# Seven half-size products per pair of hidden chunks in a banded-attention + MLP kernel

## The reference

```python
k_sum = k.reshape(B, H, nb, block, D).max(axis=3)
v_sum = v.reshape(B, H, nb, block, D).mean(axis=3)
...
a = np.exp(scores_all)
a = a / (np.sum(a, axis=-1, keepdims=True) + 1e-09)
...
g = x @ w_gate
silu = g * (1.0 / (1.0 + np.exp(-g)))
val = x @ w_val
return (silu * val @ w_out).astype(np.float32)
...
h = x @ w_in
g = np.where(pos, h, np.where(neg, 0.0, (h + beta) ** 2 / (4.0 * beta)))
return (g @ w_out).astype(np.float32)
```

## Time and profile before

| | us |
|---|---|
| median of 3 runs | 649.57 |
| lowest, highest | 646.45, 650.25 |
| span of the profiled execution | 649.1 |
| TensorE busy in it | 627.6 |
| VectorE, ScalarE, GpSimd busy | 356.3, 323.3, 30.4 |

### The profile page before, as it was taken

One profiled execution on the slowest core, in us unless ns is written; L12 is line 12 of the kernel. 1 busy time (PEld: TensorE's weight loads), 2 busy tenths in 40 slices (PEclk: granted clock), 3 DMA queues, 4 the chain that ended last, 5 costly groups with the idle time before them and its releaser, 6 DMA issues.

```text
span 649.1 us, 9400 instructions
## 1 busy us (share of the span) xinstructions
PE 627.6 (97%) x3144; PEld 510.9 (79%) x3144; DVE 356.3 (55%) x553; ACT 323.3 (50%) x622; POOL 30.4 (5%) x33
## 2 busy tenths in 40 slices
PE   5779989999999999999999999999999999999997
PEld 2648868888888888888888888888888888888885
DVE  6855455544455555445333447666666666666664
ACT  1844576773468686434333344444444444444442
POOL 3310000100010101000000000000000000000000
PEclk9989979999999999999999999999999999999999
DMA  9997936512922221322332223232253332333221
GB/s 282 261 308 215 223 98 149 160 54 99 253 97 70 75 88 57 97 98 97 97 97 97 65 66 97 97 97 97 97 164 97 97 97 97 125 134 97 97 81 65
DMA packets 49780, 78.51 MB, mean 121 GB/s; under 512 B 16481, under 2 KB 21601, under 8 KB 49505
## 3 DMA queue, kind: packets, MB, share of 16 engines
q1 hardware_dynamic: 49760, 78.27, 39.8%
HBM read 72.48 MB, written 3.15 MB: 117 GB/s over the span
## 4 chain that ended last, share of the span: by engine, by line
PE 88%; SPq 5%; DMA 3%; DVE 1%; ACT 1%; issue 1%; DVEq 0%; ACTq 0%
PE bank L409 49%; PE bank L472 20%; PE bank L454 14%; DMA v_tok<-v_rows_dram 2%; PE bank L344 2%; PE bank L335 2%; SPq L207 2%; DMA win_raw<-w_dram 1%; SPq L203 1%; PE bank L328 1%; PE bank L321 1%; SPq L226 1%; DVE k_sum L681 1%; SPq L233 0%; ACT prob L536 0%
## 5 line engine op out<-in xcount | busy, mean ns | idle before, releaser
L409 PE MATMUL bank<-x_hi,win_hi 128*128 128x512 f32 (+1 forms) x480 | 191.6, 399 | 0.0
L409 PE MATMUL bank<-x_lo,win_hi 128*128 128x512 f32 (+1 forms) x480 | 188.1, 392 | 0.0
L409 PE MATMUL bank<-x_hi,win_lo 128*128 128x512 f32 (+1 forms) x480 | 187.8, 391 | 0.0
L593 ACT ACTIVATE hid_hi<-v_tok 128x512 fp32r<-128x512 f32 x84 | 53.0, 631 | 128.4 <-DVE v_tok L804 75.5
L409 PEld LDWEIGHTS bank<-x_lo,win_hi 128*128 128x128 f32 x480 | 90.7, 189 | 19.4
L409 PEld LDWEIGHTS bank<-x_hi,win_hi 128*128 128x128 f32 x480 | 90.7, 189 | 19.2 <-issue 0.2
L409 PEld LDWEIGHTS bank<-x_hi,win_lo 128*128 128x128 f32 x480 | 90.7, 189 | 18.3 <-issue 0.2
L774 DVE TENSOR_TENSOR hid_lo<-v_tok,hid_hi 128x512 fp32r<-128x512 f32 x84 | 65.5, 780 | 56.1 <-ACT hid_hi L593 56.0
L764 DVE TENSOR_TENSOR win_lo<-win_raw,win_hi 128x512 fp32r<-128x512 f32 (+1 forms) x84 | 76.9, 916 | 19.5 <-ACT win_hi L569 19.5
L472 PE MATMUL bank<-wout_hi,hid_hi 128*128 128x512 f32 x192 | 74.8, 389 | 0.3 <-ACT hid_hi L593 0.3
L472 PE MATMUL bank<-wout_hi,hid_lo 128*128 128x512 f32 x192 | 74.8, 390 | 0.0
(11 more groups left out here) (54 smaller groups left out, 576.4 us busy)
## 6 DMA issues: line engine op xcount, KB each, us to landing
wout_raw<-w_dram SPq DMA_DIRECT2D x84, 256.0 KB, 2.6
win_raw<-w_dram SPq DMA_DIRECT2D x36, 512.0 KB, 4.1
win_raw<-w_dram SPq DMA_DIRECT2D x48, 256.0 KB, 3.0
k_slot<-k_t_dram SPq DMA_DIRECT2D x24, 192.0 KB, 4.7
v_slot<-v_rows_dram SPq DMA_DIRECT2D x24, 192.0 KB, 5.2
v_tok<-v_rows_dram SPq DMA_DIRECT2D x4, 768.0 KB, 8.9
out_dram<-v_slot SPq DMA_DIRECT2D x12, 256.0 KB, 3.0
k_raw<-k_t_dram SPq DMA_DIRECT2D x2, 1056.0 KB, 12.1
```

The costliest lines, as they stand in the source:

```text
L409: last = nc.tensor.matmul(dst[:], a, m, start=k == 0 and i == 0, stop=k == KD - 1 and i == 2)
L593: nc.scalar.activation(hid_hi[:, r], hid[:, r], ACT.Copy).then_inc(hid_hi_ready, 1)
```

## The change

**Input projections.** The tokens are taken in two groups of 768, one batch each, and each group as two halves of 384 columns (`T`). A unit makes two hidden chunks at once, as a 2 x 2 block product: the weights' blocks A11, A12, A21, A22 (two chunks by two halves of the 512 inputs) and the tokens' blocks B11, B21, B12, B22. Instead of 8 block products it makes 7 (`p1` to `p7`), with sums of blocks as operands. The sums of weights (`weight_sums`: S1 to S4) are made on GpSimd for every unit, the sums of tokens (`x_sums`: T1 to T4) once for each phase on VectorE and GpSimd. Sums are split in hi and lo like the blocks. The four outputs C11, C12, C21, C22 share partial sums: one PSUM bank (`x_ps`) collects P1, then P6, P7 and P4 on top of each other, and ScalarE copies it out after each of the first three (`p1_copy`, `u2_copy`, `u3_copy`); a second (`v_ps`) collects P5 and P3. VectorE adds a copy to a bank for C11, C22 and C12 (`c11`, `c22`, `c12`). In layer 1 a gate unit and a value unit alternate; Silu is applied to the finished copies, and GpSimd (`gated`) and VectorE (`h21`) multiply.

**Phases.** There are four: layer 1 for group 0 and for group 1, layer 2 for group 0 and for group 1, with 12, 12, 8 and 8 units. All hidden units of a phase stay in SBUF (`h`), and the output projection of the phase follows as a part of its own: `out1`, 24 matmuls of 384 columns for each of 12 chunks into 8 banks, or `out2`, 18 matmuls of 512 columns for each of 16 chunks into 6 banks. During it the seven operands of the next phase are split (`x_part_hi`, `x_part_lo`) and, in layer 2, the activation is made chunk by chunk (`rel_of`, `hid_of`).

**Attention.** The 12 tiles of batch 0 run ahead of the MLP, the 12 of batch 1 one for each unit of phase 0. For those GpSimd subtracts the maximum (`shift`) and ScalarE makes one exponential for the tile; VectorE sums it. Outputs of a tile are copied as fp32 into `raw`.

**Buffers and loops.** Tiles lie at offsets written by hand, many on top of each other; raw weights have three buffers. `wout_lo` is made by GpSimd. There are no hardware loops left.

**TensorE**, input projection: before, a step of layer 1 is a row of these three, eight times over (`x_hi,win_hi` and so on are the two operands).

The diff, cut to its core:

```diff
-            def project(dst, r, c0, tok):
-
-                for k in range(KD):
-                    c = c0 + k * P
-                    w = (win_hi[:, r, c:c + P], win_lo[:, r, c:c + P])
-                    x = (x_hi[:, k, bass.ds(tok, TB)], x_lo[:, k, bass.ds(tok, TB)])
-                    for i, (a, m) in enumerate(passes(w, x)):
-                        last = nc.tensor.matmul(dst[:], a, m, start=k == 0 and i == 0,
-                                                stop=k == KD - 1 and i == 2)
-                return last
...
+T = S // 2
+PH_LEN = (CH1, CH1, CH2 // 2, CH2 // 2)
+PH_U0 = (0, CH1, 2 * CH1, 2 * CH1 + CH2 // 2)
+CH_LEN = (CH1, CH1, CH2, CH2)
+CH_N0 = (0, CH1, 2 * CH1, 2 * CH1 + CH2)
+PHASES = 4
+UNITS = PH_U0[-1] + PH_LEN[-1]
+RAWS = 3
...
+def chunk_at(k, i):
+    return i // 2 + (i % 2) * (CH_LEN[k] // 2)
...
+            def product(dst, u, a, m, start):
+                w = u % 2
+                for kk in range(2):
+                    wh, wl = w_hi[:, w, a, kk], w_lo[:, w, a, kk]
+                    for i, (lhs, rhs) in enumerate(((wh, x_hi[:, m, kk]), (wl, x_hi[:, m, kk]), (wh, x_lo[:, m, kk]))):
+                        last = nc.tensor.matmul(dst, lhs, rhs, start=start and kk == 0 and i == 0,
+                                                stop=kk == 1 and i == 2, skip_group_check=not start)
+                return last
...
+            def p1(u):
+                k, r = phase_of(u)
+                pe.wait_ge(wa_lo, u + 1)
+                x_needed(u, 1)
+                if r >= 2 or (k == 3 and r == 1):
+                    pe.wait_ge(*c21_read(u - 2))
+                elif k:
+                    pe.wait_ge(*evacuated(k - 1, 3 * r))
+                elif r == 0:
+                    pe.wait_ge(v_sum_ready, 1)
+                else:
+                    pe.wait_ge(masked_ready, LAST_A)
+                product(x_ps(u), u, W_A11, X_B11, True).then_inc(p1_done, 1)
...
+            def p6(u):
+                x_needed(u, 3)
+                pe.wait_ge(ws_lo, u + 1)
+                pe.wait_ge(p1_copied, u + 1)
+                product(x_ps(u), u, W_S2, X_T2, False).then_inc(p6_done, 1)
...
+            def p5(u):
...
+                product(v_ps(u), u, W_S1, X_T1, True)
...
+            def p7(u):
+                x_needed(u, 5)
+                pe.wait_ge(u2_copied, u + 1)
+                product(x_ps(u), u, W_S3, X_T3, False).then_inc(p7_done, 1)
+
+            def p4(u):
+                x_needed(u, 6)
+                pe.wait_ge(wb_lo, u + 1)
+                pe.wait_ge(u3_copied, u + 1)
+                product(x_ps(u), u, W_A22, X_T4, False).then_inc(p4_done, 1)
+
+            def p3(u):
+                x_needed(u, 7)
+                pe.wait_ge(c22_ready, u + 1)
+                product(v_ps(u), u, W_S4, X_B22, False).then_inc(p3_done, 1)
...
+            for k in range(PHASES):
+                u1 = PH_U0[k] + PH_LEN[k] - 1
+                for r in range(PH_LEN[k]):
+                    u = PH_U0[k] + r
+                    late = k == 0
+                    if u >= 2:
+                        p1(u)
+                        p2(u)
+                    if late and 1 <= r < LAST_A - 1:
+                        late_scores(LAST_A + 1 + r)
+                    if r:
+                        p4(u - 1)
+                    p6(u)
+                    if late:
+                        late_transposes(LAST_A + r)
+                    if r:
+                        p3(u - 1)
+                    p5(u)
+                    if late and r == 0:
+                        late_scores(LAST_A + 1)
+                    p7(u)
+                    if late:
+                        values(LAST_A + r, tile_out(AT1))
+                if k < 2:
+                    out1(k, 0, (0, 1, 2, 4, 6, 7))
+                    p3(u1)
+                    p4(u1)
+                    out1(k, 0, (5, 3)).then_inc(out_done, 1)
+                    for i in range(1, CH_LEN[k]):
+                        out1(k, i, range(len(ACC1)), ends=i == CH_LEN[k] - 1).then_inc(out_done, 1)
+                else:
+                    out2(k, 0).then_inc(out_done, 1)
+                    p4(u1)
+                    p3(u1)
+                    for i in range(1, CH_LEN[k]):
+                        out2(k, i, ends=i == CH_LEN[k] - 1).then_inc(out_done, 1)
...
+                    hh, hl = hid_hi[:, r, j * P:j * P + P], hid_lo[:, r, j * P:j * P + P]
+                    for e, (lhs, rhs) in enumerate(((hh, wout_hi[:, r]), (hh, wout_lo[:, r]), (hl, wout_hi[:, r]))):
+                        if j == 0 and e == 0:
+                            pe.wait_ge(hid_hi_ready, n + 1)
+                            pe.wait_ge(wout_lo_ready, n + 1)
+                        if j == 0 and e == 2:
+                            pe.wait_ge(hid_lo_ready, n + 1)
+                        last = nc.tensor.matmul(bank[ACC2[j]][:], lhs, rhs, start=i == 0 and e == 0,
+                                                stop=ends and e == 2)
...
+            def p1_copy(u):
+                act.wait_ge(p1_done, u + 1)
+                part_free(u, c11_ready, 1)
+                nc.scalar.activation(part[:, u % 2, 0], x_ps(u), ACT.Copy).then_inc(p1_copied, 1)
...
+            def wout_part_hi(k, i):
+                n, _ = block_of(k, i)
+                act.wait_ge(wout_loaded[n % RAWS], 16 * (n // RAWS + 1))
+                if n >= 2:
+                    act.wait_ge(out_done, n - 1)
+                nc.scalar.activation(wout_hi[:, n % 2], wout_raw[:, n % RAWS], ACT.Copy).then_inc(wout_hi_ready, 1)
...
+            def rel_of(k, i):
+                n, c = block_of(k, i)
+                m = n - CH_N0[2]
+                act.wait_ge(c12_ready, PH_U0[k] + i // 2 + 1)
+                if m >= 2:
+                    act.wait_ge(g_ready, m - 1)
+                nc.scalar.activation(rel[:, n % 2], h[:, c], ACT.Relu, scale=0.5, bias=half[:, 0:1]
+                                     ).then_inc(rel_ready, 1)
...
+                for i in range(1, CH_LEN[k]):
+                    wout_part_hi(k, i)
+                    hid_part_hi(k, i)
+                    if k >= 2:
+                        if i == 1:
+                            take_c21(u1)
+                        if i < CH_LEN[k] - 1:
+                            rel_of(k, i + 1)
+                    if k < PHASES - 1:
+                        if 2 <= i < 9:
+                            x_part_hi(k + 1, i - 2)
...
+            def hid_of(k, i):
+                n, c = block_of(k, i)
+                m = n - CH_N0[2]
+                dve.wait_ge(rel_ready, m + 1)
+                nc.vector.scalar_tensor_tensor(rel[:, n % 2], rel[:, n % 2], 1.0, rel[:, n % 2], ALU.min, ALU.mult
+                                               ).then_inc(sq_ready, 1)
+                dve.wait_ge(sq_ready, m + 1)
+                nc.vector.tensor_tensor(h[:, c], h[:, c], rel[:, n % 2], ALU.max).then_inc(g_ready, 1)
...
+                for i in range(1, CH_LEN[k]):
+                    if k >= 2 and i < CH_LEN[k] - 1:
+                        hid_of(k, i + 1)
+                    if i > 1:
+                        hid_part_lo(k, i)
+                    if k < PHASES - 1:
+                        if i == 1:
+                            x_sums(k + 1)
+                        elif i < 9:
+                            x_part_lo(k + 1, i - 2)
...
+            def weight_sums(u):
+                w = w_raw[:, u % RAWS]
+                a11, a12, a21, a22 = w[:, 0, 0:2], w[:, 0, 2:4], w[:, 1, 0:2], w[:, 1, 2:4]
+                s2, s1, s3, s4 = (w_sum[:, i] for i in range(4))
+                pool.wait_ge(w_loaded[u % RAWS], 32 * (u // RAWS + 1))
+                if u:
+                    pool.wait_ge(ws_lo, u)
+                nc.gpsimd.tensor_tensor(s1, a21, a22, ALU.add).then_inc(s_step, 1)
+                nc.gpsimd.tensor_tensor(s3, a11, a21, ALU.subtract)
+                pool.wait_ge(s_step, 2 * u + 1)
+                nc.gpsimd.tensor_tensor(s2, s1, a11, ALU.subtract).then_inc(s_step, 1)
+                pool.wait_ge(s_step, 2 * u + 2)
+                nc.gpsimd.tensor_tensor(s4, a12, s2, ALU.subtract).then_inc(s_ready, 1)
...
+            first_inverses(LAST_A - 1)
+            first_copy_out(6)
+            w_lo_a(0)
+            first_copy_out(7)
+            x_part_lo(0, X_B11)
+            x_part_lo(0, X_B21)
+            mask_scores(LAST_A, quads(AT0))
+            first_copy_out(8)
+            w_lo_a(1)
+            first_copy_out(9)
+            w_lo_s(0)
+            w_lo_b(0)
+            first_copy_out(10)
+            late_inverses(LAST_A)
+            first_copy_out(11)
+            x_sums(0)
+            x_part_lo(0, X_T2)
+            c11(0)
```

1347 lines of the change are left out of this document (801 added, 546 removed).

## The result

The changed kernel takes 685.05 us (median of 4 runs, 682.35 to 686.59); the kernel before, run beside it, 648.03 (646.45 to 650.25). The ratio is 1.056 (95% interval 1.053 to 1.059): slower by 37 us, and outside the predicted range of 624 to 661.

The account below looks back on a forecast made before the run. TensorE's matmul stream plus its holes was taken as the bound. 77.7 (start) + (521.8 + 27.6 - 10.6) + 1.6 + 18 (output phases) + 3 + 1.5 + 3.4 = 644 us, against a 649.1 span; 8-in-10 range 624 to 661.

Parts of the forecast that it names:

- Part 1: TensorE's matmuls: 384 columns take 173.4 ns, so the stream is 521.8 us, 33.2 less; ends 514 and 566.
- Part 2: The start: third product of unit 0 near 72.5 us; +19.6 us, against -9.2 for fewer late tiles; ends 6 either way.
- my 25.3: At the start, VectorE's passes one after another from tile 8's mask on, with one 0.9 wait: 25.3 us.
- Part 3: Second layer's output phases: waits at every second chunk and at the heads cost 18 us together; ends 0 and 30.
- 5.6 us chain: Second layer's output phases: from chunk i-2's last matmul through ScalarE and VectorE to chunk i's third matmul, 5.6 us.
- 9.0 us pair: Second layer's output phases: two chunks take 9.0 us in place of 8.16, costing 5.1 us a phase.
- Part 4: GpSimd beside VectorE: 3 us for holes in units and phase heads, ends 0 to 14, plus 1.5 for lower clock.
- 3.2 in parts 2 and 3: Lumps for GpSimd: 2 us of waiting at the start, 1.2 us in the first of the second layer's output phases.
- slack of 1.2 us: Late units of 9.6 us: the chain from scores through mask, `shift`, exponential, inverse and `normalise` to transposes keeps 1.2 us.
- The slower one: VectorE and GpSimd in turns pace late units, +1.9 us each, +4 in the first `hid_of` phase: 657, up to 670; 0.17.
- Neither faster rival: Output phases don't wait: 626 us, 0.20; or 384 columns take 170.0 ns or less and start loads land sooner: 633, 0.15.
- The signs of being wrong: Prediction is wrong if the second layer's phases show TensorE without holes, or late units take over 10.5 us.

Follow-up runs that it names:

- Experiment 2: On the changed kernel, loads that wait for nothing put ahead of `v_sum`, and tile 8's ahead of the second `v_tok`: 677.67 us, ratio 1.043.
- Experiment 5: On the changed kernel, ScalarE's `rel_of(i+1)` put ahead of `wout_part_hi(i)` in the second layer's output phases: 672.28 us, ratio 1.039.
- 4: On the changed kernel, `wout_part_lo` of all 56 chunks on VectorE in place of GpSimd: 681.01 us, ratio 1.050.
- Experiment 7: On the changed kernel, GpSimd's `weight_sums`, `wout_part_lo` and first-phase `x_sums` mostly cut to 8 elements, so other numbers are computed: 662.25 us, ratio 1.022.
- experiment 10: On the changed kernel, late softmax without GpSimd's `shift` and VectorE's sum (four ScalarE passes), GpSimd's first `x_sums` behind VectorE's second: 681.93 us, ratio 1.052.
- 8: On the changed kernel, the new load order, `rel_of` ahead, `u3_copy` ahead of `late_exp`, and `hid_of(2)` ahead of `hid_part_lo(1)`: 659.61 us, ratio 1.019.
- 9: The kernel of experiment 8 without `u3_copy` first, with `x_sums` and phase 2's x parts placed at later chunks: 662.33 us, ratio 1.021.

## Why the prediction was wrong

**Part 1 (matmuls) was right.** 173.3 ns against 173.4, between the ends 170.0 and 193. The Trainium skill's 2.5 ns (TensorE: Matmul & The Clock Gate, "Wait — 56ns, not 53.3ns?") would have given 162.5; two sizes here, 512 and 384 columns, both show 13.4, so the measurement decides.

**Part 2 (the start) was mis-sized by 12.6 us, outside its ends of 6.** Half of it, 6.3, is the arrival of tile 8: 51.29 in place of 45. I divided bytes by a rate of the kernel before; the trace shows tile 8's loads issued at 34.99 behind the second `v_tok`, with 5.60 and 4.38 us for its queries and its keys where the issues before took 1.1 to 2.9, and the queue idle from 15.15 to 23.35, where `load_v_sum(0)` waits. Experiment 2 takes 7 us off by order alone (by the medians). The other 6.3 is from tile 8's scores to the third product, 33.8 us in place of 27.5. The scores came at half clock (0.50 granted from 51 to 53, behind the 13.1 us in which TensorE stood), and VectorE's first mask 2.1 us behind them. From there, first the length of the stretch and the busy time of TensorE, its weight loads, VectorE, ScalarE and GpSimd with their instructions, the granted clock, the DMA share and GB/s, then VectorE's two longest waits:

```profile
53.38:85.06 31.68, 23.70 (x241) 17.95 (x239) 25.89 (x45) 18.23 (x51) 14.24 (x13) 0.93 0.60 159
```
```profile
DVE w_lo L1019 <- ACT w_hi L760: 2.0, 2, 1.5
DVE x_lo L1014 <- ACT x_hi L753: 1.5, 2, 0.9
```

VectorE is busy 25.9 us (24.4 forecast: my 25.3 held a wait of 0.9; and 2.3 of the 25.9 is blocking in the two rows of 79.86 and 83.21), and idle 5.8, where I had 0.9 and 2.

**Part 3 was right in mechanism and short in size.** The 5.6 us chain and the 9.0 us pair came out (5.6 and 9.14). Experiment 5 takes the chain away and the hole goes; experiments 4 and 7 take GpSimd's passes away and it stays. The first layer's output was forecast to cost nothing; it had holes of 1.6 and 1.1 us a phase, by `wout_part_lo` behind `x_sums` and `weight_sums` on GpSimd's queue, which I had not followed. The head of the first hid_of phase was forecast at 3.3 us more, and was 7.3, plus 2.2 at half clock (to the next chunk's start at 478.79); that of the last phase was 4.1, plus some 1.6. With the holes behind the head, the two phases lost 33.2 us where 18 were forecast (144.5 and 135.7 against 123.55).

**Part 4 is the step that failed.** "I book 3 us for holes", with passes at their undisturbed length elsewhere in the sum, though the row of 86.06 showed a pass standing for most of the common time and I quoted it. Experiment 7 puts a price of 20 to 23 us on most passes of three of the five jobs that GpSimd got, where 3 were booked here and 3.2 in parts 2 and 3. How much of it is blocking and how much GpSimd's own queue stays open. The lock runs in both directions, which that one row did not show, so GpSimd's own passes lengthen too (1042 ns before; `shift` 1448, `wout_lo` 1519), and with them the late tiles' chain. Its slack of 1.2 us was used up and late units took 10.1 us (9.44 without the three helpers' passes; 9.44 and 9.82 without `shift`, experiment 10).

**The rivals.** The slower one had the mechanism, at 0.17 with 657 and at most 670. It was the true one, priced per unit (+1.9 against 11.5 us; the units came to 10.1) and too cheap in the output phases (+4), where most of it fell. Neither faster rival held. The price was a mean; a blocked pass at a place where TensorE is waiting costs what it is lengthened by, and off the path (experiment 5) nothing.

**The signs of being wrong** didn't show it. The second layer's phases had holes, and past the first two units (10.7 and 10.6) no late unit took over 10.2; both were set on parts whose mechanism held, and neither on the size of the start or of the heads.

What stays open: how much of the start's 12.6 us is VectorE's waiting and how much the queue's, since experiments 2, 8 and 9 show third products from 74.3 to 81.8 with the same load order, one profiled execution each.

## What to carry to other kernels

When a change puts work on GpSimd beside a VectorE that does two-input passes, add the two engines' passes as on one engine at every place where TensorE waits for either, and look for places where three or four such passes meet. Passes for later work should stand one at a time between passes that are waited for, not in a block behind them: the same products took 685 us in the order of the change, and 638 with the loads, ScalarE's and VectorE's lists in another order, the work for the next group spread out, and two jobs (`shift` and most of `wout_lo`) taken off GpSimd. An arithmetic saving of 33 us was real, and was worth 11 once the order was right.

## What the runs showed of the hardware

- A matmul in fp32r, in a stretch at the upper clock, takes its columns at 2.4 GHz plus 13.4 ns at 384 and at 512 columns alike (173.3 and 226.7 ns).
- GpSimd and VectorE passes with two SBUF inputs exclude each other both ways, an in-place pass on one tensor (`rel`) too: 0.96 becomes 2.56 us (465.89) beside a GpSimd pass of 768 elements, which itself takes 2.5 (465.15). Even a GpSimd pass of 8 elements (0.20 us alone) took 0.97 us behind a VectorE pass of 0.96 (experiment 7, 79.69 beside 79.65).
- A VectorE pass with one input from PSUM isn't touched: `part<-bank` took 0.55 us in the middle of a GpSimd pass (84.92, beside 84.15 to 85.90), and as a mean it takes the same 0.55 here and in experiment 7. So the trace agrees with the Trainium skill there too (SBUF — State Buffer, "Who interferes with whom").

```profile
84.15 1.75 POOL L1207 TENSOR_TENSOR prob<-prob,inv 128x512 f32<-128x512 f32 x1
84.92 0.55 DVE L1038 TENSOR_TENSOR part<-bank,part 128x384 f32<-128x384 f32 x1
```
